# A first routed tile of the fullest expert worked off in the tail of the dense part, with that expert at place 0 of the order

## The reference

```python
kv = np.einsum('bhsd,bhse->bhde', k, v)
out = np.einsum('bhsd,bhde->bhse', q, kv)
...                                        # root mean square norm, gain
p = domain_probs / (domain_probs.sum(-1, keepdims=True) + 1e-09)
for e in range(4):                         # every token through all 4 experts, w1 512x1024, w2 1024x512
    h = np.maximum(x @ w1[e], 0.0)
    out += p[:, e:e + 1] * (h @ w2[e])
...
logits = xn @ en.T / tau                   # 8 experts, each token to the best one
expert_idx = np.argmax(logits, axis=1)
for e in range(8):
    mask = expert_idx == e
    h = np.maximum(x[mask] @ w1[e], 0.0)
    out[mask] = gate_w[mask, None] * (h @ w2[e])
```

## Time and profile before

| | us |
|---|---|
| median of 3 runs | 1148.67 (1148.01 to 1149.37) |
| the profiled execution, its own time | 1150.23 |
| span of that execution, first to last instruction | 1148.6 |
| PE busy / DVE / ACT / POOL | 1120.3 / 724.8 / 456.1 / 655.2 |
| mean granted TensorE clock, share of 2.4 GHz | 0.993 |

### The profile page before, as it was taken

The page is one execution under the profiler, slowest core; times in us unless marked ns, Lnnn a source line. Parts: engine busy times, 40 slices in busy tenths (PEclk is TensorE's granted clock), DMA queues, the critical chain, the costliest instruction groups (busy, mean ns, idle before and its releaser), DMA issues.

```text
span 1148.6 us, 18710 instructions
## 1 busy us (share of the span) xinstructions
PE 1120.3 (98%) x6210; PEld 985.3 (86%) x6211; DVE 724.8 (63%) x1160; ACT 456.1 (40%) x812; POOL 655.2 (57%) x609
## 2 busy tenths in 40 slices
PE   8899999999999999999999999999989999999996
PEld 7888999988889888988889888998887888888885
DVE  4777888888875868888875878888662222222221
ACT  4683444444534444444534444444222222222220
POOL 1487777799868777799868777777330111111101
PEclk9999999999999999999999999999989999999998
DMA  9956778777712348877712348777369759327960
GB/s 231 253 137 195 261 276 281 280 261 261 252 37 74 120 152 303 287 261 258 252 37 74 121 164 303 276 272 276 134 252 379 279 185 372 151 103 300 377 235 13
DMA packets 102433, 250.87 MB, mean 218 GB/s; under 512 B 8254, under 2 KB 48190, under 8 KB 94171
## 3 DMA queue, kind: packets, MB, share of 16 engines
q1 hardware_dynamic: 97360, 235.18, 59.7%
q0 software_dynamic: 4800, 14.72, 3.7%
q10 hardware_dynamic: 203, 0.05, 0.0%
HBM read 170.99 MB, written 79.98 MB: 218 GB/s over the span
## 4 chain that ended last, share of the span: by engine, by line
PE 81%; DVE 5%; POOL 5%; DMA 3%; issue 3%; ACT 2%; SPq 0%; ACTq 0%; DVEq 0%; POOLq 0%
PE ps L1285 25%; PE ps L1287 25%; PE ps L1286 25%; PE ps L1495 2%; DMA w_raw<-in_moe_w_dram 1%; POOL w_lo L486 1%; DVE x_rows L972 1%; PE ps L1243 1%; PE ps L1461 1%; DMA q<-in_q_dram 1%; POOL dispatched_rows L551 1%; DMA probs_rows<-in_moe_domain_probs_dram 1%; DVE hT_lo L961 1%; DVE x_ops_lo L985 0%; POOL w_lo L481 0%
## 5 line engine op out<-in xcount | busy, mean ns | idle before, releaser
L1285 PE MATMUL ps<-x_ops_hi,w_hi 128*128 128x384 f32 x672 | 227.1, 338 | 5.4 <-DVE sum L942 3.2
L1285 PE MATMUL ps<-w_hi,hT_hi 128*128 128x512 f32 x576 | 226.8, 394 | 0.0
L1287 PE MATMUL ps<-x_ops_hi,w_lo 128*128 128x384 f32 x672 | 225.8, 336 | 0.0
L1287 PE MATMUL ps<-w_hi,hT_lo 128*128 128x512 f32 x576 | 225.2, 391 | 0.0
L1286 PE MATMUL ps<-w_lo,hT_hi 128*128 128x512 f32 x576 | 225.0, 391 | 0.0
L1286 PE MATMUL ps<-x_ops_lo,w_hi 128*128 128x384 f32 x672 | 225.0, 335 | 0.0
L972 DVE SCALAR_TENSOR_TENSOR x_rows<-ps,dense_probs,x_rows 128x512 f32<-128x512 f32 x270 | 189.9, 738 | 17.9 <-PE ps L1287 17.8
L611 POOL DMA_INDIRECT out_dram<-y_rows,row_ids x22 | 22.6, 1026 | 236.3 <-DVE y_rows L1176 141.8
L495 POOL TENSOR_TENSOR w_lo<-w_raw,w_hi 128x512 fp32r<-128x512 f32 x96 | 148.8, 1570 | 8.0 <-ACT w_hi L705 8.0
L1166 DVE TENSOR_TENSOR rhT_lo<-ps,rhT_hi 128x512 fp32r<-128x512 f32 x44 | 28.4, 686 | 172.0 <-ACT rhT_hi L831 172.0
L1285 PEld LDWEIGHTS ps<-x_ops_hi,w_hi 128*128 128x128 f32 x672 | 126.1, 188 | 11.0 <-DVE sum L942 5.1
(11 more groups left out here) (204 smaller groups left out, 1993.5 us busy)
## 6 DMA issues: line engine op xcount, KB each, us to landing
w_slots<-split_parts SPq DMA_DIRECT2D x64, 1024.0 KB, 5.6
w_raw<-in_moe_w_dram SPq DMA_DIRECT2D x96, 512.0 KB, 3.6
ahead_raw<-in_moe_w_dram SPq DMA_DIRECT2D x64, 512.0 KB, 6.7
split_parts<-ahead_hi SPq DMA_DIRECT2D x64, 512.0 KB, 4.1
split_parts<-ahead_lo SPq DMA_DIRECT2D x64, 512.0 KB, 5.7
row_tile<-dispatched_rows POOLq DMA_DIRECT2D x20, 257.0 KB, 5.7
kv<-in_k_dram SPq DMA_DIRECT2D x16, 288.0 KB, 8.3
kv<-in_v_dram SPq DMA_DIRECT2D x16, 288.0 KB, 8.6
```

The costliest lines, as they stand in the source:

```text
L1285: mm(out_, ah, bh, start=(first and m == 0), stop=False, skip_group_check=not final or not first)
L1287: last = mm(out_, al, bh, start=False, stop=(final and m == n - 1), skip_group_check=not final or not first)
```

## The change

1. **Which expert.** In step 46, DVE finds from the counts after the first four blocks the expert with the most rows so far (`find_star`, 18 small instructions in five parts between the adds of that step). It changes places with expert 0: place 0 is the fullest expert, and expert 0 stands at that expert's place. The other tables get this exchange too (4 instructions more before `tab_r`, 3 more for `tab_e`). With the reference's inputs the fullest is expert 3, so places 0 to 7 have 6, 5, 2, 1, 2, 1, 3 and 2 tiles.
2. **Early tile.** The first 128 rows of that expert are its tile 0, complete since step 38. SP loads them before the tail. PE flips them behind the second pair of the tail (n == 1), ACT and DVE split them there. PE's up and down of this tile (48 matmuls) and its hidden flips stand around the last routing and in front of the table's reader. The three groups of filler matmuls (24, 4 and 6) are gone. DVE splits the tile's hidden values by halves (`rt_half`) inside the code of the tables.
3. **Loads.** In the tail, SP loads w1 of the star expert, its first two w2 pieces into the slots of the next expert's w1, and two pieces of the next expert; after the dense part, the other two w2 pieces; after the rows, the first two w2 pieces again, into their own slots; after the early tile, what is left of the next expert. These are 18 pieces where there were 16.
4. **First pair apart.** Tiles 0 and 1 stand in front of the loops of all engines, which begin at 1.

```diff
@@ SP @@
-            sp.wait_ge(up_done, OPS * STEPS)
+            sp.wait_ge(star_ready, 2)
+            e_star = sp.value_load(tab_s[0:1, 0:1], min_val=0, max_val=E2 - 1)
+            e_next = sp.value_load(tab_s[0:1, 1:2], min_val=0, max_val=E2 - 1)
+            r_star = sp.value_load(tab_s[0:1, 2:3], min_val=P, max_val=E2 * CAP)
...
+            sp.wait_ge(scattered, 16 * T0)
+            sp.dma_start(xs[:, 0, :], rows[bass.ds(r_star, P), :]).then_inc(first_rows_in[0], 16)
+            sp.wait_ge(up_done, OPS * STEPS)
+            for c in range(2):
+                load_piece(c, e_star, 0, c)
+            for c in range(2):
+                load_early(PCS + 2 + c, c)
+            for c in range(2):
+                sp.wait_ge(part_in[0][c], 16)
+                load_piece(2 + c, e_star, 0, 2 + c)
+            for c in range(2):
+                sp.wait_ge(part_in[0][c], 32)
+                load_piece(PCS + c, e_next, 0, c)
...
+            sp.wait_ge(ry_done, 2)
+            for c in range(2, PCS):
+                sp.wait_ge(part_in[0][c % 2], 48)
+                load_piece(PCS + c, e_next, 0, c)
@@ DVE @@
+            def find_star(part):
+
+                if part == 0:
+                    dve.wait_ge(rank_read, NB - 3)
+                    step(V.tensor_tensor(ecol[:, 0, :], run[:, :], ebase[:, :], ALU.subtract))
+                    step(V.tensor_reduce(star_col[:, 0:1], ecol[:, 0, :], AX.X, ALU.max))
...
+                if part == 2:
+                    step(V.scalar_tensor_tensor(swap[:, :], knum[:, 0:E2], 0.0, star[:, :], ALU.is_equal, ALU.subtract))
+                    step(V.scalar_tensor_tensor(ecol[:, 2, :], swap[:, :], star_col[:, 2:3], knum[:, 0:E2], ALU.mult, ALU.add))
...
+                        if k == STAR_AT and j < 5:
+                            find_star(j)
...
+                if n == 2:
+                    rx(0, 0)
+                    V.tensor_copy(early_gi[:, :], xs[:, 0, D:D + 2]).then_inc(gi_copied, 1)
...
             step(V.tensor_tensor(ec(0), run[:, :], ebase[:, :], ALU.subtract))
+            step(V.tensor_tensor(ec(1), ec(0), star[:, :], ALU.mult))
+            step(V.tensor_reduce(star_col[:, 0:1], ec(1), AX.X, ALU.add))
+            step(V.tensor_tensor(star_col[:, 1:2], star_col[:, 0:1], ec(0)[:, 0:1], ALU.subtract))
+            step(V.scalar_tensor_tensor(ec(0), swap[:, :], star_col[:, 1:2], ec(0), ALU.mult, ALU.add))
...
+            rt_half(0, 0, 0)
@@ PE @@
+                if t == T0:
+                    pe.wait_ge(rx_split, 1)
...
             for n, (kk, j) in enumerate(TAIL):
                 down(kk, j)
+                if n == 1:
+                    pe.wait_ge(h_lo, 4 * LAST + 1)
+                    flip_rows(0, 0)
...
             logits(TT - 1, LAST)
+            early_up(0, (0, 1, 2))
             ranks(NB - 1, LAST)
...
+            early_up(0, (3,))
+            early_up(1, (0, 1))
+            pe.wait_ge(rank_read, NB)
+            flip_half(0, 0)
+            early_up(1, (2, 3))
+            early_down((0, 1))
+            flip_half(0, 1)
+            early_down((2, 3))
+            early_down((4, 5))
...
-            for _ in range(2 * WARM):
-                mm(ps[:, 6, 0:P], ident[:, :], ident[:, :], start=True, stop=True)
             pe.wait_ge(tab_ready, 2)
-            for _ in range(WARM // 3):
-                mm(ps[:, 6, 0:P], ident[:, :], ident[:, :], start=True, stop=True)
             tiles = pe.value_load(tab_n[0:1, 0:1], min_val=TT, max_val=KT)
-            flip_rows(0, 0)
-            for _ in range(WARM // 2):
-                mm(ps[:, 6, 0:P], ident[:, :], ident[:, :], start=True, stop=True)
             flip_rows(1, 1)
-            routed_up(0, 0)
-            flip_hidden(0)
-            with pe.Fori(0, PAIRS) as i:
+            early_down((6, 7))
+            flip_rows(2, 0)
+            routed_up(1, 1)
+            flip_hidden(1)
+            flip_rows(3, 1)
+            routed_up(2, 0)
```

More of the change, by code:

```diff
@@ L188, in build @@
     two = keep("two_first", [P, E2])
+    star = keep("star", [P, E2])
+    swap = keep("star_swap", [P, E2])
+    star_col = keep("star_cols", [P, 4])
+    starts = keep("place_starts", [P, E2])
+    jumps = keep("place_jumps", [P, E2])
+    kstart = keep("tile_ends", [P, TAB])
+    tab_s = keep("table_star", [P, 3], I32)
+    early_gi = keep("early_gate_and_id", [P, 2])
     tab_o = keep("table_place_of_tile", [P, TAB], I32)
@@ L613, in store @@
                                      bounds_check=NTOK - 1, oob_is_err=False).then_inc(stored[s], 16)
-            with pool.Fori(0, PAIRS) as i:
+            for s in range(2):
+                store(s, s)
+                pool.wait_ge(rx_done, s + 3)
+                pool.wait_ge(gi_copied, s + 3)
+                load_rows(s + 4, s)
+            with pool.Fori(1, PAIRS) as i:
                 with pool.If(2 * i < tiles):
@@ L810, in _, with rx, relu_half, rt_half @@
                         exponentials(b)
-            for t in range(TT - TPT, TT):
+            def rx(n, s):
+                act.wait_ge(rx_done, n + 1)
+                A(rxh[:, s, :], ps[:, 7 * s, :], ACT.Copy).then_inc(rx_hi, 1)
+            def relu_half(n, half):
+                act.wait_ge(rh_done, 2 * n + half + 2)
+                A(hs[:, half * 512:(half + 1) * 512], ps[:, 1 + half, :], ACT.Relu).then_inc(rh_relu, 1)
+            def rt_half(n, s, half):
+                act.wait_ge(rt_done, 2 * n + half + 1)
+                A(rhh[:, s, half * 512:(half + 1) * 512], ps[:, 3 + half, :], ACT.Copy).then_inc(rt_hi, 1)
+            def relu_rows(n):
+                for half in range(2):
+                    relu_half(n, half)
+            def rt_parts(n, s):
+                for half in range(2):
+                    rt_half(n, s, half)
+            for s in range(2):
+                act.wait_ge(s_out[s], 32 * (NAHEAD // 2))
+            rx(0, 0)
+            for t in range(T0, TT):
                 route(t)
@@ L816, in _ @@
             exponentials(NB - 1)
[L819 to L835 removed]
+            for half in range(2):
+                relu_half(0, half)
+                rt_half(0, 0, half)
             act.wait_ge(tab_ready, 2)
             tiles = act.value_load(tab_n[0:1, 0:1], min_val=TT, max_val=KT)
[L838 removed]
             rx(1, 1)
[L840 to L842 removed]
+            rx(2, 0)
+            relu_rows(1)
+            rt_parts(1, 1)
+            rx(3, 1)
+            relu_rows(2)
+            rt_parts(2, 0)
+            with act.Fori(1, PAIRS) as i:
                 with act.If(2 * i < tiles):
@@ new lines, in rx, with rt_half @@
+            def rx(n, s):
+                dve.wait_ge(rx_hi, n + 1)
+                V.tensor_tensor(rxl[:, s, :], ps[:, 7 * s, :], rxh[:, s, :].bitcast(F32), ALU.subtract).then_inc(rx_split, 1)
+            def rt_half(n, s, half):
+                dve.wait_ge(rt_hi, 2 * n + half + 1)
+                V.tensor_tensor(rhl[:, s, half * 512:(half + 1) * 512], ps[:, 3 + half, :],
+                                rhh[:, s, half * 512:(half + 1) * 512].bitcast(F32), ALU.subtract).then_inc(rt_split, 1)
@@ L1490, in flip_hidden @@
                 for half in range(2):
-                    pe.wait_ge(rh_relu, 2 * n + half + 1)
-                    for c in range(4):
-                        m = half * 512 + c * P
-                        last = tr(ps[:, 3 + half, c * P:(c + 1) * P], hs[:, m:m + P], ident[:, :])
-                    last.then_inc(rt_done, 1)
+                    flip_half(n, half)
             def routed_down(n, s, wh, e, off):
```

213 lines of the change are left out of this document (133 added, 80 removed).

## The result

| | us |
|---|---|
| changed kernel, median of 6 runs | 1153.19 (1148.40 to 1154.97) |
| kernel before, median of 6 runs beside them | 1148.21 (1146.83 to 1149.37) |
| ratio, 95% interval | 1.0037 (1.0024 to 1.0050) |
| the profiled execution of the changed kernel, its own time and span | 1148.40 and 1146.8 |

The change makes the kernel slower, by 4.2 us by the ratio (the medians are 5.0 apart), where I had forecast 1.5 us faster. The execution that was profiled is the shortest of the six.

A forecast was written before the change was run, and what follows sets the result against it. PE, busy 98% of the span, was taken as the bound, with one large hole between dense and routed parts. Head -9.2 plus hole at up(17) +7.7 gave -1.5 us from 1148.67: 1147.2, range 1142.3 to 1151.8.

The forecast's parts named there:

- The head: Way into the routed part: the early tile fills PE's hole, gaining 9.2 us, 10.6 if the clock stays up, about 7.5 if low.
- up(3) at 887.1: Start of tile 3's up on PE: 887.1 instead of 896.30; the prediction is wrong if outside 885 to 889.
- the ranks 2.2 us late: Last ranks, behind nine early-tile matmuls: 2.2 us late at a clock low until about 852, 0.8 late at full clock.
- the first rows: Row tiles landing after the tables: rows land at 863.9, and PE waits 0.7 us for the second row tile.
- the way from up(1) to up(3): PE's first routed tiles: 20.8 us in the new order instead of 25.04, with some 0.5 for POOL's late row tile.
- The place and the cause of the hole: At up(17), behind small places: PE waits for `w_slots`, as three matrices load back to back from about 1025.
- The size of the hole: At up(17): three matrices take 34.5 us, first pair 5.2 late; costs 7.7 us, 5.8 to 13.4 by pace.
- The clock in the hole: At up(17): a falling clock costs 0, or 2.8 us if low for the other 12 matmuls as well.
- The sum: Whole kernel: head -9.2 plus hole +7.7 makes -1.5 us, 1147.2 on the median.
- the rival of slow loads: At up(17): slow loads, pace above 12.8 us a matrix; at 13.41 the hole is 13.4, time 1152.9; chance 0.12.
- The clock at the head: Before the routed part: clock fell after some 3 us of flips and logits, then idling; low about 3.4 us, not 7.
- The rule weighed: Loads ahead of up(17): at about 358 GB/s a matrix takes 13.1 us, the hole is 12.5, the time 1152.0.

The follow-up runs named there:

- after_again: The changed kernel run again with no edit, for more runs and a second profile (1152.68 us): median 1152.27 us, ratio 1.0036 to the kernel before.
- before_rotated: The kernel before with experts numbered 3, 0, 1, 2, 4, 5, 6, 7, as a control: 1149.38 us, ratio 1.0012 to the kernel before.
- after_half_w2: The changed kernel loading only the first half of the columns of each w2 piece from place 2 on: 1150.96 us, ratio 1.0018 to the kernel before.
- after_deep: The changed kernel with four pieces of weights in flight instead of two: 1147.01 us, ratio 0.9986 to the kernel before.
- after_rot_deep: The changed kernel with places of 6, 1, 5, 2, 2, 1, 3, 2 tiles and four pieces in flight: 1141.59 us, ratio 0.9945 to the kernel before.
- Experiment 2: Experts renumbered: changed kernel without three small places in a row, 1141.54 us; kernel before with that numbering, 1149.38; kernel before with experts 0 and 3 exchanged, 1161.63.

## Why the prediction was wrong, by its steps

- **The head: right for the two profiles of the change.** I said 9.2 us, and 10.6 if the clock stays up. Measured were 8.3 with the clock low for 3.4 us and 9.8 with it up: each term 0.8 or 0.9 too large. up(3) at 887.1 was 883.9, outside my own 885 to 889, or 886.5 once the 2.6 us of the dense part are put back; in `after_again` it was 885.4. In detail: the ranks 2.2 us late with a low clock and 0.8 late without were 2.4 and 0.9 (by the time from SP's first load; 27.18 us in the kernel before); the wait of 1.6 for the first hidden split was 1.53. `find_star` costs nothing that these traces show: SP's first load comes at 819.8 to 821.2 in the profiles of the changed kernel and its variants that had no low clock early in the dense part, and at 821.18 in `before_rotated`. What I had too late were the first rows (no wait, where I had 0.7), and what I had too small is the way from up(1) to up(3), 21.6 us for 20.8, with a wait of 0.72 for a row tile of POOL. What I had not counted on is a second stretch of low clock at about 874: `after_half_w2`, `after_deep` and `after_rot_deep` have it, with heads of 66.4, 66.8 and 66.5 us, a gain of only some 6 where I had 7.5 as the least. How often the changed kernel itself has it, two profiles can't tell.
- **The place and the cause of the hole: right.** up(17), its first matmul, three matrices back to back from the moment that down(12) frees the slots. The anchor is exact: 1025.0 - 887.1 is 137.9, and 1021.81 - 883.89 is 137.9. Experiment 2 puts it in and takes it out.
- **The size of the hole: the step that failed.** "Three matrices take 10.87 + 12.27 + 11.4 = 34.5", and the first pair 8.04 after that. It was 11.43 + 11.68 + 14.27 = 37.4 and 8.1 in one execution, 11.54 + 11.76 + 13.27 = 36.6 and 11.1 in the other. 42.5 us became 45.5 and 47.6, and the hole of 7.7 became 10.7 and 13.5. I took the pace from matrices that had time, from a stretch with full engines, though the same rows had one of 13.41 us with 295 GB/s. My pace of 11.5 us for a matrix is that of full engines: `after_deep`, with four pieces in flight, has 11.3 and a hole of 7.6. That 7.6 is so near my 7.7 is in part chance, since each of its pieces takes 10.8 us to land. What was missing is what two pieces in flight lose against that, 3 to 6 us.
- **The clock in the hole: 0, as I took it.** In the changed kernel the clock fell within the wait (0.86 in 1064 to 1065) and the first matmuls ran at 0.63 us each; all 12 were done before the second pair landed. That is why the thirteenth waited only 0.28 us (0.99 in `after_again`) and not 2.5. The other bound exists too: in `after_half_w2` the clock fell later, and its hole was 9.2 us (1062.84 to 1084.54, less 12.52), 3.2 more than its waits.
- **The sum.** -9.2 + 7.7 became -8.3 + 13.5 = +5.2 for an execution like the second profile and -9.8 + 10.7 = +0.9 for the first; the ratios say +4.2 and +4.1, the medians +5.0 and +4.9. This is the rival of slow loads, to which I gave 0.12: its place and its price (13.4) came true. Its condition did not, as I had put it: a matrix took 12.2 to 12.5 us on average and not over 12.8, and the late first pair, 11.1 us in the second profile, made up the rest. The range ended at 1151.8 because I gave the pace of 13.41 too little weight.
- **The clock at the head.** I read the rows as a clock that fell when PE had done flips and logits and then stood still. It was already 0.72 in 848 to 849 of before, with the last logits ending at 848.53. In `after_again` it fell from 846 on (0.68 in 846 to 847) with matmuls right behind the logits, and in the first profile of the change, with the same work, it did not fall. So these traces do not show what makes it fall.
- **The rule weighed.** The Trainium skill, DMA: Bandwidth & Descriptors, Specifications, with its 358 GB/s gave 1152.0, close to the result, but not for its reason: the trace shows 401 GB/s over 24 us of the changed kernel and 419 in `after_deep`. The 295 GB/s of 897 to 911, which I had read as near it, stood with engines busy for 0.85, so they are no limit. The same page of the Trainium skill, Bandwidth, says that its measurements, for loads issued from GpSimd, were made on a single core with the pair's other core idle, and lists 341 GB/s for one transfer of 1 MB and 425 for 16 MB. That fits the 401 to 426 GB/s of these windows better, though no trace here shows what the other core did.

What stays open is why single pieces land late (9.0 us for the one issued at 1049.91, with a median of 6.1 in 1024 to 1066). It is not their number in flight alone, which was the same ahead of it, and the hole's size differs by 2.8 us between two executions of one kernel. POOL's row tile issued at 1049.61 was late as well, 8.1 us with a median of 6.2; whether one delayed the other, no run tests.

## What to carry to other kernels

When a change reorders groups that are loaded through a double buffer, sum the loads behind each run of small groups against the work that hides them; a place that the change seems to leave alone can cost more than its aim gains. Give the worst row of the trace its weight in the pace of such a run, beside the loads that had slack, and ask how much of it is bytes: read the DMA share and the GB/s of each window together, against the best window of the same loads. Here a share under 1, or less GB/s at a full share, stood where four transfers in flight gained; with both at their best, another order was what was left. And take a second profile before explaining a median: the one execution that I read first was 4.8 us from it.
